# The last stage's output products with the weight as stationary operand and 512 tokens moving, in a fused recurrence and feed-forward kernel on one Trainium2 core

## The chip, the cores and the metric

The kernel runs on one core of a Trainium2 chip. The metric is the device time of one execution in microseconds (us), the median over several runs. The core's engines are called as the profile calls them: PE is TensorE (matrix products), PEld its weight loads, DVE is VectorE, ACT is ScalarE, POOL is GpSimd, and SP is the engine whose queue issues the DMAs.

## The reference

Three parts follow each other: a linear recurrence with decay over 768 positions (2 batches, 8 heads of 48), a mixture of four experts on the 1,536 tokens, and a last feed-forward stage. Only the last is touched:

```python
def _moe2_ref(x, w_in, w_out) -> np.ndarray:      # x 1536 x 384, w_in 384 x 2048, w_out 2048 x 384
    h = x @ w_in
    g = h * (1.0 / (1.0 + np.exp(-1.702 * h)))
    return (g @ w_out).astype(np.float32)
```

## The kernel before, in words

All activations between the parts are kept on the chip with the 384 model features as rows, in three tiles of 128 partitions (`KT` = 3), and the tokens as columns. Every product is made three times to keep float32 precision: an operand is split into a high part that the PE reads exactly and a low remainder, and high x high, high x low and low x high are added up in PSUM (`PASSES`). So each logical product of 128 x 128 x columns is three matmuls.

The expert part and the last stage are one list of steps. A step j is 128 hidden features of one stage for one block of tokens (512 tokens; the first four blocks of expert 0 have 256). `hidden(j)` (L909) makes these 128 hidden features: three k-tiles by three passes, nine matmuls with the input weight stationary and the tokens of `x_hi` or `x_lo` moving. `output(j)` multiplies the hidden features by the output weight and adds to the block's output in PSUM. In the expert part (L931) that is also nine matmuls: for each of three tiles of 128 output features, the weight is stationary and the tokens of `h_hi` or `h_lo` move. In the last stage (L946) it is turned round: for each of four tiles of 128 tokens (`t`), the hidden features are stationary and the 384 columns of the output weight move, so that the output has its tokens as rows, as the reference wants it. That is twelve matmuls.

The last stage has 48 steps: three blocks of 512 tokens, 16 steps each (`STEPS1` is the number of the first). PE's order is written out: hidden(j), then output(j-2), from the third step of the stage on; at the end the last two outputs stand behind each other. Between hidden and output of a step ACT and DVE work in turns: ACT takes the sigmoid of the hidden features (L581, into `acc`), DVE multiplies (L740), ACT rounds the result to the high part `h_hi` (L583), DVE makes the low part `h_lo` (L742). `hidden(j)` waits until the hidden bank of step j-2 was read, `output(j)` waits for `h_lo` of its step. ACT waits for the outputs of step j-3 before it overwrites its slot of `h_hi` (a ring of three).

The finished outputs of a block are copied out of PSUM by ACT (`store_block`, L562), one copy for each tile of 128 tokens. In ACT's order they come before the sigmoid of the block's step 18 (two steps into the next block), and for the last block at the very end. A copy waits for the semaphore `tile`, which PE raises after each of a block's last products but the final one, and for `l2` for the final one; the copies go into `out_sb`, a ring of `OUT_RING` pieces in the tensor `p_bc`, and SP stores each to the output in DRAM (L412) as it is done. The PSUM banks of the outputs are two sets of three (`OUT_SETS`, 0 to 2 and 5 to 7); four token tiles a block walk through both sets (`out_bank2`).

Of the kernel before, what the change touches and what calls it, by code (L numbers as in the profile page):

```python
# [31 lines left out]
F32 = mybir.dt.float32  # L32
F32R = mybir.dt.float32r
U32 = mybir.dt.uint32
ACT = mybir.ActivationFunctionType

P = 128
# [3 lines left out]
N = B * S  # L41
DM = H * D
# [5 lines left out]
KT = DM // P  # L48
NB = 512
BLOCKS = N // NB  # L50
# [9 lines left out]
MOE_BLOCKS = len(SPANS)  # L60
# [6 lines left out]
SCALED = [64, 32, 16, 8, 4, 2]  # L67
XBUF = 3
HRING = 3
OUT_RING = 4  # L70
MID = P // 2
W_LEAST, W_MOST = 0.5, 1.5
AT_RING = 3
# [4 lines left out]
def build(nc, rkT, rkvN, w_rows, w_flat, u_flat, probs, weights, out):  # L78
    p_dram = nc.dram_tensor("p_normalised", [E, N], F32, kind="Internal").ap()
    ctx = ExitStack()  # L80
    with ctx:
# [10 lines left out]
        sem = {}  # L92
# [11 lines left out]
        s_prob = [ctx.enter_context(nc.semaphore(f"s_prob{i}")) for i in range(2)]  # L104
        s_store = [ctx.enter_context(nc.semaphore(f"s_store{i}")) for i in range(OUT_RING)]

        def sb(stack, name, shape, dt=F32):
            return stack.enter_context(nc.sbuf_tensor(name, shape, dt))
# [7 lines left out]
        bank = ctx.enter_context(nc.psum_tensor("bank", [P, 8, 512], F32))  # L116
# [13 lines left out]
        p_bc = [sb(ctx, "p_bc0", [P, N]), None]  # L130
# [41 lines left out]
        sig = [acc[:, 0, 0:NB], acc[:, 1, 0:NB]]  # L172
        gated = [acc[:, 2, 0:NB], acc[:, 0, NB:2 * NB]]

        out_sb = [p_bc[0][:, i * DM:(i + 1) * DM] for i in range(OUT_RING)]


        w_row, w_ok = part[0:1, 0, 0:H * D], part[0:1, 1, 0:H * D]
# [12 lines left out]
        OUT_SETS = ((0, 1, 2), (5, 6, 7))  # L191

        def out_tile(n, k):


            if n < SMALLS:
                return bank[:, 5 + k // 2, k % 2 * SMALL:(k % 2 + 1) * SMALL]
            return bank[:, OUT_SETS[n % 2][k], :]

        def out_bank2(m):  # L200

            return OUT_SETS[m // KT % 2][m % KT]

        def spans(ap, m):

# [10 lines left out]
        def where(j):  # L216

            if j < STEPS1:
                n, f = divmod(j, FT)
                t, size = SPANS[n]  # L220
                return expert_of(n), f, slice(t, t + size), f == 0, f == FT - 1
            b, f = divmod(j - STEPS1, F2 // P)
            return E + f // FT, f % FT, slice(b * NB, (b + 1) * NB), f == 0, f == F2 // P - 1
# [20 lines left out]
        def part_of(tensors, f, piece):  # L244
            t = tensors[piece]
            if piece:
                return t[:, f * DM:(f + 1) * DM]
            return t[:, :].rearrange("p (k n) -> p k n", k=KT)[:, :, f * P:(f + 1) * P]
# [44 lines left out]
        def _(sp):  # L293
# [9 lines left out]
            def load_stage(s):  # L303
                for i in range(2):
                    sp.dma_start(staging[i][:, :], weights[2 * s + i]).then_inc(s_stage[i], 16)
# [101 lines left out]
                load_stage(e + 1)  # L407
            sp.wait_ge(sem["wlo"], 2 * FT * E)
            load_stage(STAGES - 1)
            for n in range(BLOCKS * NB // P):  # L410
                sp.wait_ge(sem["ev2"], n + 1)
                sp.dma_start(out[n * P:(n + 1) * P, :], out_sb[n % OUT_RING]).then_inc(s_store[n % OUT_RING], 16)  # L412
            for i in range(OUT_RING):
                sp.wait_ge(s_store[i], 16 * (BLOCKS * NB // P // OUT_RING))


        @block.gpsimd
# [91 lines left out]
        def _(act):  # L509
# [40 lines left out]

            def store_block(b):

                for t in range(NB // P):
                    m = b * (NB // P) + t

                    if t < NB // P - 1:
                        act.wait_ge(sem["tile"], b * (NB // P - 1) + t + 1)
                    else:
                        act.wait_ge(sem["l2"], STEPS1 + (b + 1) * F2 // P)
                    if m >= OUT_RING:  # L560
                        act.wait_ge(s_store[m % OUT_RING], 16 * (m // OUT_RING))
                    act.activation(out_sb[m % OUT_RING], bank[:, out_bank2(m), 0:DM], ACT.Copy).then_inc(sem["ev2"], 1)  # L562

            def step(j):
                g = j - STEPS1
# [56 lines left out]
            with act.Else():  # L622
                for u in range(UNITS):
                    c, p = divmod(u, PAIRS)
# [20 lines left out]
            for j in range(JOIN, STEPS):  # L645
                step(j)
            store_block(BLOCKS - 1)


# [221 lines left out]
        def _(pe):  # L871
            pe.wait_ge(sem["ident"], 2)
            pe.wait_ge(sem["wr"], 1)
            for p in range(PAIRS):
                last = pe.transpose(table_t[:, p * P:(p + 1) * P], w_rev[:, p, :], ident[:, :])
# [4 lines left out]
            xs, hs = (x_hi, x_lo), (h_hi, h_lo)  # L880
# [3 lines left out]
            def wait_weights(s, f, piece):  # L884
                if s == 0:
                    pe.wait_ge(sem["wlo0"], STAGE0.index((f, piece)) + 1)
                else:
                    pe.wait_ge(sem["wlo"], 2 * FT * (s - 1) + 2 * f + piece + 1)
# [25 lines left out]
            def output(j):  # L914

                s, f, tokens, first, last_f = where(j)
                size = tokens.stop - tokens.start
                slot = j % HRING
                if tokens.start == 0:
                    wait_weights(s, f, 1)  # L920
                pe.wait_ge(sem["hlo"], j + 1)
                if j < STEPS1:
                    n = j // FT
                    if first and 1 <= n < SMALLS:
                        pe.wait_ge(sem["ev1"], KT * n)
                    if first and n > SMALLS:
                        pe.wait_ge(sem["ev1"], KT * (n - 1))
                    for k in range(KT):
                        for i, (a, c) in enumerate(PASSES):
                            w = part_of(w_parts[a][s % 2], f, 1)  # L930
                            last = pe.matmul(out_tile(n, k), w[:, k * P:(k + 1) * P], hs[c][:, slot, 0:size],  # L931


                                             start=(first and i == 0 and not (n < SMALLS and k == 1)),
                                             stop=(last_f and i == 2 and (n >= SMALLS or k > 0)))
                else:
                    for t in range(NB // P):
                        m = tokens.start // P + t
                        if first:
                            if m < 2 * KT:  # L940
                                pe.wait_ge(sem["ev1"], KT * (MOE_BLOCKS - 2) + m + 1)
                            else:
                                pe.wait_ge(sem["ev2"], m - 2 * KT + 1)
                        for i, (a, c) in enumerate(PASSES):
                            w = part_of(w_parts[a][s % 2], f, 1)
                            last = pe.matmul(bank[:, out_bank2(m), 0:DM], hs[c][:, slot, t * P:(t + 1) * P], w,  # L946
                                             start=(first and i == 0), stop=(last_f and i == 2))
                        if last_f and t < NB // P - 1:
                            last.then_inc(sem["tile"], 1)
                last.then_inc(sem["l2"], 1)  # L950

# [2 lines left out]
            with pe.If(quick == 1):  # L954
# [46 lines left out]
                for what, i in SCHEDULE:  # L1001
                    if what == "unit":
                        unit(i)
                    elif what == "weigh":
                        weigh(i)
                    elif what == "hidden":
                        hidden(i)
                    elif what == "output":
                        output(i)
            with pe.Else():  # L1010
                def level(dst, col, g, m, p, c):

                    rows = slice(g * HP, (g + 1) * HP)
                    x, o = c % XBUF, c % 2
                    width = 64 if m == 64 else P
                    if m == 1:
                        key, rec = k_in[rows, x, p, :], r_in[rows, x, p, 1:P:2]
                    else:
                        n = SCALED.index(m)
                        key, rec = G["k_lev"][rows, o, n, p, 0:width], G["r_lev"][rows, o, n, p, :]  # L1020
                    return pe.matmul(dst[0:width, g, col:col + HP], key, rec, start=True, stop=True)
# [20 lines left out]
                for u in range(UNITS):  # L1042
                    c, p = divmod(u, PAIRS)
# [8 lines left out]
                    for n, m in enumerate(HIGH):  # L1052
                        for g in range(2):
                            last = level(G_HIGH, n * HP, g, m, p, c)
# [3 lines left out]
                    for n, m in enumerate(LOW):  # L1058
                        for g in range(2):
                            last = level(G_LOW, n * HP, g, m, p, c)  # L1060
                    last.then_inc(sem["g_low"], 1)
                    if ci < CPB - 1:
                        if updates(u) > 1:
                            pe.wait_ge(sem["g_st"], updates(u) - 1)
                        for g in range(2):
                            last = pe.matmul(G_KV[LIVE[g], 0:D], kn_in[:, c % XBUF, (2 * p + g) * D:(2 * p + g + 1) * D],
                                             v_in[:, c % XBUF, 2 * p + g, :], start=True, stop=True)
# [5 lines left out]
                for what, i in GENERAL:  # L1073
                    if what == "hidden":
                        hidden(i)
                    elif what == "output":
                        output(i)
            for j in range(JOIN, STEPS):
                hidden(j)
                if j <= STEPS1:  # L1080
                    output(j - 1)
                if j >= STEPS1 + 2:
                    output(j - 2)
# [51 lines left out]
```

## Time and profile before

| | us |
|---|---|
| median of 3 runs | 704.76 |
| lowest and highest | 704.3, 707.44 |
| span of the profiled execution, first to last instruction | 702.7 |
| PE busy | 682.2 (97%) |
| DVE, ACT, POOL busy | 240.9, 215.4, 180.0 |
| last stage, first output matmul (504.92) to the last matmul's end (699.75) | 194.8 |

For the profiled execution the span is known and not its device time; the median lies 2.1 us above the span. Busy time of PE counts a matmul from its start to its modelled end, and these overlap (a matmul is shown with 0.33 to 0.40 us and the next one starts 0.17 to 0.23 us behind it), so what a matmul costs in a stream is read from start to start.

### The profile page before, as it was taken

The numbers are of one execution on the slowest core, as the hardware profiler recorded it, in microseconds if no ns is written. First come the engines' busy times: TensorE is split into PE (matmuls) and PEld (weight loads), VectorE is DVE, ScalarE is ACT, GpSimd is POOL, SyncE is SP. The second block draws the span as 40 slices with busy tenths as digits, with TensorE's granted clock in tenths as the row PEclk, the third lists the DMA queues.
The fourth block names the chain that finished last, engine by engine and source line by source line (L and its number), as shares of the span: only waits on it lengthen the run. The fifth ranks groups of instructions, "written<-read, shape, count | busy, mean of one in ns | idle before, by whom it ended". The sixth has DMA issues, their size and how long they took to land.

```text
span 702.7 us, 9199 instructions
## 1 busy us (share of the span) xinstructions
PE 682.2 (97%) x3636; PEld 563.4 (80%) x3636; DVE 240.9 (34%) x433; ACT 215.4 (31%) x455; POOL 180.0 (26%) x172
## 2 busy tenths in 40 slices
PE   3899999999999999999999999999999999999998
PEld 1457778778888888888888888888899999999997
DVE  7666755432131212121213223121443333333332
ACT  4245532332332221122221122322453232323223
POOL 5424242200532423032422043532292000000000
PEclk9999999999999999999999999999999999999999
DMA  7253462101032004010004000021000010001001
GB/s 278 83 209 128 132 250 72 65 5 52 1 122 104 0 1 165 15 46 0 1 1 179 1 1 0 1 105 75 0 1 1 1 46 0 1 1 45 1 1 45
DMA packets 11987, 39.24 MB, mean 56 GB/s; under 512 B 3233, under 2 KB 6050, under 8 KB 10658
## 3 DMA queue, kind: packets, MB, share of 16 engines
q1 hardware_dynamic: 11938, 38.60, 15.1%
q8 instruction: 30, 0.49, 0.3%
q14 instruction: 19, 0.16, 0.1%
HBM read 35.61 MB, written 2.38 MB: 54 GB/s over the span
## 4 chain that ended last, share of the span: by engine, by line
PE 95%; DVE 3%; issue 1%; ACT 0%; DMA 0%; DVEq 0%
PE bank L909 42%; PE bank L931 28%; PE bank L946 14%; PE bank L984 3%; PE bank L970 2%; PE bank L967 2%; PE bank L993 1%; DVE q_r_mid L760 1%; DVE q_k_mid L757 1%; DVE q_a_t L768 0%; DVE q_tab_k L661 0%; DMA w_sb<-w_rows 0%; DVE w_pow L656 0%; DVE psum_sb L685 0%; DVE psum_sb L687 0%
## 5 line engine op out<-in xcount | busy, mean ns | idle before, releaser
L909 PE MATMUL bank<-x_hi,w_hi 128*128 128x512 f32 (+1 forms) x480 | 178.2, 371 | 1.5 <-issue 1.5
L909 PE MATMUL bank<-x_hi,w_lo 128*128 128x512 f32 (+1 forms) x480 | 177.8, 370 | 0.0
L909 PE MATMUL bank<-x_lo,w_hi 128*128 128x512 f32 (+1 forms) x480 | 177.7, 370 | 0.0
L732 DVE SCALAR_TENSOR_TENSOR h_lo<-bank,h_hi 128x512 fp32r<-128x512 f32 (+1 forms) x112 | 68.9, 615 | 295.6 <-ACT h_hi L575 295.6
L575 ACT ACTIVATE h_hi<-bank 128x512 fp32r<-128x512 f32 (+1 forms) x112 | 60.1, 537 | 314.0 <-PE bank L909 314.0
L485 POOL TENSOR_TENSOR w_lo<-staging,w_hi 128x384 fp32r<-128x384 f32 x80 | 82.1, 1038 | 174.3 <-ACT w_hi L537 174.3
L931 PE MATMUL bank<-h_hi,w_hi 128*128 128x512 f32 (+1 forms) x336 | 123.0, 366 | 1.3 <-DVE acc L722 1.3
L931 PE MATMUL bank<-h_lo,w_hi 128*128 128x512 f32 (+1 forms) x336 | 120.4, 358 | 0.0
L931 PE MATMUL bank<-h_hi,w_lo 128*128 128x512 f32 (+1 forms) x336 | 120.4, 358 | 0.0
L909 PEld LDWEIGHTS bank<-x_hi,w_hi 128*128 128x128 f32 x480 | 90.8, 189 | 17.5 <-issue 3.3
L909 PEld LDWEIGHTS bank<-x_hi,w_lo 128*128 128x128 f32 x480 | 90.8, 189 | 15.1
L909 PEld LDWEIGHTS bank<-x_lo,w_hi 128*128 128x128 f32 x480 | 90.8, 189 | 14.0
L931 PEld LDWEIGHTS bank<-h_hi,w_hi 128*128 128x128 f32 x336 | 63.1, 188 | 15.3 <-issue 5.2
L931 PEld LDWEIGHTS bank<-h_lo,w_hi 128*128 128x128 f32 x336 | 63.2, 188 | 9.5
L931 PEld LDWEIGHTS bank<-h_hi,w_lo 128*128 128x128 f32 x336 | 63.2, 188 | 9.3
L740 DVE TENSOR_TENSOR acc<-bank,acc 128x512 f32<-128x512 f32 x48 | 33.2, 692 | 94.7 <-ACT acc L581 94.7
L946 PE MATMUL bank<-w_lo,h_hi 128*128 128x384 f32 x192 | 64.8, 337 | 0.0
L946 PE MATMUL bank<-w_hi,h_hi 128*128 128x384 f32 x192 | 64.6, 337 | 0.0
L946 PE MATMUL bank<-w_hi,h_lo 128*128 128x384 f32 x192 | 64.5, 336 | 0.0
L581 ACT ACTIVATE acc<-bank 128x512 f32<-128x512 f32 x48 | 28.6, 596 | 89.1 <-PE bank L909 89.1
L494 POOL TENSOR_TENSOR acc<-acc,part 128x512 f32<-128x512 f32 x27 | 34.2, 1293 | 84.9 <-DVE part L722 84.9
L537 ACT ACTIVATE w_hi<-staging 128x384 fp32r<-128x384 f32 x96 | 47.4, 515 | 0.9 <-DMA staging<-weights 0.9
(67 smaller groups left out, 553.3 us busy)
## 6 DMA issues: line engine op xcount, KB each, us to landing
staging<-weights SPq DMA_DIRECT2D x10, 1536.0 KB, 8.6
rkv_in<-rkv_n SPq DMA_DIRECT2D x12, 576.0 KB, 4.6
rk_in<-rk_t SPq DMA_DIRECT2D x12, 512.0 KB, 3.8
staging<-weights SPq DMA_DIRECT2D x4, 768.0 KB, 8.9
p_bc<-p_normalised SPq DMA_DIRECT2D x4, 768.0 KB, 5.1
out<-p_bc SPq DMA_DIRECT2D x12, 192.0 KB, 2.0
y_sb<-y_sb SPq DMA_DIRECT2D x72, 8.0 KB, 1.8
u_bc<-u_flat SPq DMA_DIRECT2D x1, 192.0 KB, 6.0
```

The lines of the kernel that those rows point to most:

```text
L485: pool.tensor_tensor(part_of(w_lo[s % 2], f, piece), part_of(staging, f, piece), part_of(w_hi[s % 2], f, piece).bitcast(F32), ALU.subtract ...
L494: pool.tensor_tensor(acc[:, k, cols], acc[:, k, cols], part[:, i % 2, :], ALU.add).then_inc(sem["acc"], 1)
L537: act.activation(part_of(w_hi[s % 2], f, piece), part_of(staging, f, piece), ACT.Copy).then_inc(sem["whi"], 1)
L575: act.activation(h_hi[:, j % HRING, 0:size], hid, ACT.Relu).then_inc(sem["hhi"], 1)
L581: act.activation(sig[g % 2], hid, ACT.Sigmoid, scale=1.702).then_inc(sem["sig"], 1)
L732: dve.scalar_tensor_tensor(h_lo[:, slot, 0:size], hid, 0.0, h_hi[:, slot, 0:size].bitcast(F32), ALU.max, ALU.subtract).then_inc(sem["hlo"], 1)
L740: dve.tensor_tensor(gated[g % 2], hid, sig[g % 2], ALU.mult).then_inc(sem["gate"], 1)
L909: last = pe.matmul(bank[:, HID[j % 2], 0:tokens.stop - tokens.start], w[:, k, :], xs[c][:, k, tokens], start=(n == 0), stop=(n == 3 * KT - 1))
L931: last = pe.matmul(out_tile(n, k), w[:, k * P:(k + 1) * P], hs[c][:, slot, 0:size],   start=(first and i == 0 and not (n < SMALLS and k == ...
L946: last = pe.matmul(bank[:, out_bank2(m), 0:DM], hs[c][:, slot, t * P:(t + 1) * P], w, start=(first and i == 0), stop=(last_f and i == 2))
L967: pe.matmul(y_of(Y_BANK, g, p), state[rows, ci % 2, p, :], r_in[rows, x, p, :], start=True, stop=False)
L984: pe.matmul(bank[:, A_BANKS[u % 2], 0:2 * P], k_mid[:, o, p, :], r_mid[:, o, p, :, :], start=True, stop=True).then_inc(sem["q_a"], 1)
```

## The change

The output products of the last stage take the form of the expert part. For each of three tiles of 128 output features (`k`) the weight's 128 columns are stationary and all 512 tokens of `h_hi` or `h_lo` move, nine matmuls a step instead of twelve. The output of a block lies in one set of three banks, features as rows, 512 tokens as columns. `store_block` makes three copies of 128x512 instead of four of 128x384, SP issues nine stores of 256 KB instead of twelve of 192 KB, each into 128 rows of 2,048 bytes of an output tensor that is 384 x 1,536. The ring `out_sb` has three pieces of 512 columns instead of four of 384, so each copy from the second block on also waits for the store of one block before. The final transposition is made on the host.

```diff
-OUT_RING = 4
+OUT_RING = 3
+STORES = BLOCKS * KT
-        out_sb = [p_bc[0][:, i * DM:(i + 1) * DM] for i in range(OUT_RING)]
+        out_sb = [p_bc[0][:, i * NB:(i + 1) * NB] for i in range(OUT_RING)]
-            for n in range(BLOCKS * NB // P):
-                sp.wait_ge(sem["ev2"], n + 1)
-                sp.dma_start(out[n * P:(n + 1) * P, :], out_sb[n % OUT_RING]).then_inc(s_store[n % OUT_RING], 16)
+            for m in range(STORES):
+                b, k = divmod(m, KT)
+                sp.wait_ge(sem["ev2"], m + 1)
+                sp.dma_start(out[k * P:(k + 1) * P, b * NB:(b + 1) * NB], out_sb[m % OUT_RING]).then_inc(s_store[m % OUT_RING], 16)
 def store_block(b):
-                for t in range(NB // P):
-                    m = b * (NB // P) + t
-                    if t < NB // P - 1:
-                        act.wait_ge(sem["tile"], b * (NB // P - 1) + t + 1)
+                for k in range(KT):
+                    m = b * KT + k
+                    if k < KT - 1:
+                        act.wait_ge(sem["tile"], b * (KT - 1) + k + 1)
...
-                    act.activation(out_sb[m % OUT_RING], bank[:, out_bank2(m), 0:DM], ACT.Copy).then_inc(sem["ev2"], 1)
+                    act.activation(out_sb[m % OUT_RING], out_tile(MOE_BLOCKS + b, k), ACT.Copy).then_inc(sem["ev2"], 1)
 def output(j):
-                    for t in range(NB // P):
-                        m = tokens.start // P + t
+                    b = tokens.start // NB
+                    for k in range(KT):
+                        m = b * KT + k
...
-                            last = pe.matmul(bank[:, out_bank2(m), 0:DM], hs[c][:, slot, t * P:(t + 1) * P], w,
+                            last = pe.matmul(out_tile(MOE_BLOCKS + b, k), w[:, k * P:(k + 1) * P], hs[c][:, slot, :],
                                              start=(first and i == 0), stop=(last_f and i == 2))
-    out = nc.dram_tensor("out", (N, DM), F32, kind="ExternalOutput").ap()
+    out = nc.dram_tensor("out", (DM, N), F32, kind="ExternalOutput").ap()
-    return result.results[0]["out"]
+    return np.ascontiguousarray(result.results[0]["out"].T)
```

On PE, between two hidden steps of the last stage, this stood before (in a name pair the moving operand is named first for a product with a stationary weight; `w_hi,h_hi` has the weight moving):

```order
3128 L946 MATMUL bank<-w_hi,h_hi 128x384
3129 L946 MATMUL bank<-w_hi,h_lo 128x384
3130 L946 MATMUL bank<-w_lo,h_hi 128x384
3131 L946 MATMUL bank<-w_hi,h_hi 128x384
3132 L946 MATMUL bank<-w_hi,h_lo 128x384
3133 L946 MATMUL bank<-w_lo,h_hi 128x384
3134 L946 MATMUL bank<-w_hi,h_hi 128x384
3135 L946 MATMUL bank<-w_hi,h_lo 128x384
3136 L946 MATMUL bank<-w_lo,h_hi 128x384
3137 L946 MATMUL bank<-w_hi,h_hi 128x384
3138 L946 MATMUL bank<-w_hi,h_lo 128x384
3139 L946 MATMUL bank<-w_lo,h_hi 128x384
```

And on PE at the same kind of place now, with the first matmul of the next hidden step behind it (line 945 is the changed line 946, line 907 the unchanged 909):

```order
3137 L945 MATMUL bank<-h_hi,w_hi 128x512
3138 L945 MATMUL bank<-h_lo,w_hi 128x512
3139 L945 MATMUL bank<-h_hi,w_lo 128x512
3140 L945 MATMUL bank<-h_hi,w_hi 128x512
3141 L945 MATMUL bank<-h_lo,w_hi 128x512
3142 L945 MATMUL bank<-h_hi,w_lo 128x512
3143 L945 MATMUL bank<-h_hi,w_hi 128x512
3144 L945 MATMUL bank<-h_lo,w_hi 128x512
3145 L945 MATMUL bank<-h_hi,w_lo 128x512
3146 L907 MATMUL bank<-x_hi,w_hi 128x512
```

Twelve matmuls of 384 columns have become nine of 512, the same number of columns; the place in PE's order is the same.

On ACT, at the end of the program, this stood before (L581 and L583 are the sigmoid and the rounding of the last step, L562 the copies of the last block):

```order
532 L581 ACTIVATE acc<-bank 128x512
533 L583 ACTIVATE h_hi<-acc 128x512
534 L581 ACTIVATE acc<-bank 128x512
535 L583 ACTIVATE h_hi<-acc 128x512
536 L562 ACTIVATE p_bc<-bank 128x384 x4
```

And on ACT at the same place now:

```order
532 L579 ACTIVATE acc<-bank 128x512
533 L581 ACTIVATE h_hi<-acc 128x512
534 L579 ACTIVATE acc<-bank 128x512
535 L581 ACTIVATE h_hi<-acc 128x512
536 L560 ACTIVATE p_bc<-bank 128x512 x3
```

Four copies of 384 columns have become three of 512, at the same place.

## Rows read from the trace of the kernel before

**Rows 1.** The page: busy time, then granted clock over 40 slices, then the chain.

```profile
PE 682.2 (97%) x3636; PEld 563.4 (80%) x3636; DVE 240.9 (34%) x433; ACT 215.4 (31%) x455; POOL 180.0 (26%) x172
...
PEclk9999999999999999999999999999999999999999
...
PE 95%; DVE 3%; issue 1%; ACT 0%; DMA 0%; DVEq 0%
```

**Rows 2.** Two stretches: length, then busy us of PE, PEld, DVE, ACT, POOL.

```profile
300.00:400.00 100.00, 100.00 (x443) 82.79 (x442) 22.87 (x34) 20.97 (x40) 27.52 (x25) 1.00 0.11 40
513.29:597.05 83.76, 83.76 (x422) 75.90 (x421) 30.33 (x41) 30.50 (x55) 18.09 (x17) 1.00 0.03 10
```

**Rows 3.** The chain in order of time, from 492: start, us, what.

```profile
498.96 2.04 PE bank L931 x9
501.00 4.08 PE bank L909 x18
```

**Rows 4.** The same view, from 480 to the end.

```profile
509.27 2.10 PE bank L946 x12
511.37 2.08 PE bank L909 x9
...
693.48 6.28 PE bank L946 x36
```

**Rows 5.** Timeline of PE around the first last-stage output: start, duration, instruction.

```profile
504.92 0.33 PE L946 MATMUL bank<-w_hi,h_hi 128*128 128x384 f32 x1
...
505.44 0.35 PE L946 MATMUL bank<-w_hi,h_hi 128*128 128x384 f32 x1
505.63 0.34 PE L946 MATMUL bank<-w_hi,h_lo 128*128 128x384 f32 x1
505.80 0.34 PE L946 MATMUL bank<-w_lo,h_hi 128*128 128x384 f32 x1
505.99 0.33 PE L946 MATMUL bank<-w_hi,h_hi 128*128 128x384 f32 x1
...
507.02 0.39 PE L909 MATMUL bank<-x_hi,w_hi 128*128 128x512 f32 x1
```

**Rows 6.** Timeline of PE in the last output steps and of ACT beside them.

```profile
694.38 0.33 PE L946 MATMUL bank<-w_hi,h_hi 128*128 128x384 f32 x1
...
695.60 0.69 DVE L742 TENSOR_TENSOR h_lo<-acc,h_hi 128x512 fp32r<-128x512 f32 x1 [0.70 <-ACT h_hi L583]
...
699.41 0.34 PE L946 MATMUL bank<-w_lo,h_hi 128*128 128x384 f32 x1
```

**Rows 7.** Timeline of one step: ACT and DVE between two hidden steps.

```profile
689.13 0.33 PE L946 MATMUL bank<-w_hi,h_hi 128*128 128x384 f32 x1
...
689.33 0.60 ACT L581 ACTIVATE acc<-bank 128x512 f32<-128x512 f32 x1 [2.14 <-PE bank L909]
...
691.41 0.69 DVE L742 TENSOR_TENSOR h_lo<-acc,h_hi 128x512 fp32r<-128x512 f32 x1 [0.70 <-ACT h_hi L583]
```

**Rows 8.** Timeline of ACT at a block's end, then the waits from 495 on.

```profile
569.87 1.61 ACT L562 ACTIVATE p_bc<-bank 128x384 f32<-128x384 f32 x4
...
ACT acc L581 <- PE bank L909: 89.1, 45, 2.2
```

**Rows 9.** Groups of ACT from 500 on: busy us, mean ns, idle before.

```profile
L581 ACT ACTIVATE acc<-bank 128x512 f32<-128x512 f32 x47 | 28.0, 596 | 86.9 <-PE bank L909 86.9
...
L562 ACT ACTIVATE p_bc<-bank 128x384 f32<-128x384 f32 x12 | 5.2, 490 | 2.7 <-PE bank L946 2.7
```

**Rows 10.** The last instructions of ACT (chain, from 690), and the DMA issues of the page.

```profile
699.79 0.49 ACT p_bc L562
...
staging<-weights SPq DMA_DIRECT2D x10, 1536.0 KB, 8.6
...
rk_in<-rk_t SPq DMA_DIRECT2D x12, 512.0 KB, 3.8
...
out<-p_bc SPq DMA_DIRECT2D x12, 192.0 KB, 2.0
```

More of the change, by code:

```diff
@@ L198, in out_tile @@
             return bank[:, OUT_SETS[n % 2][k], :]
-        def out_bank2(m):
-            return OUT_SETS[m // KT % 2][m % KT]
         def spans(ap, m):
@@ L409, in _ @@
             load_stage(STAGES - 1)
-            for n in range(BLOCKS * NB // P):
-                sp.wait_ge(sem["ev2"], n + 1)
-                sp.dma_start(out[n * P:(n + 1) * P, :], out_sb[n % OUT_RING]).then_inc(s_store[n % OUT_RING], 16)
+            for m in range(STORES):
+                b, k = divmod(m, KT)
+                sp.wait_ge(sem["ev2"], m + 1)
+                sp.dma_start(out[k * P:(k + 1) * P, b * NB:(b + 1) * NB], out_sb[m % OUT_RING]).then_inc(s_store[m % OUT_RING], 16)
             for i in range(OUT_RING):
-                sp.wait_ge(s_store[i], 16 * (BLOCKS * NB // P // OUT_RING))
+                sp.wait_ge(s_store[i], 16 * (STORES // OUT_RING))
         @block.gpsimd
@@ L945, in output @@
                             w = part_of(w_parts[a][s % 2], f, 1)
-                            last = pe.matmul(bank[:, out_bank2(m), 0:DM], hs[c][:, slot, t * P:(t + 1) * P], w,
+                            last = pe.matmul(out_tile(MOE_BLOCKS + b, k), w[:, k * P:(k + 1) * P], hs[c][:, slot, :],
                                              start=(first and i == 0), stop=(last_f and i == 2))
-                        if last_f and t < NB // P - 1:
+                        if last_f and k < KT - 1:
                             last.then_inc(sem["tile"], 1)
```

## The prediction

> **What bounds the kernel now.** I read the page first: PE is busy 97% of the span, the chain that ended last is PE for 95% of it, and the granted clock is full (2.4 GHz) in all 40 slices [rows 1]. DVE, ACT and POOL are each busy for about a third. Next the stretches: in the last stage, 513.29 to 597.05, PE is busy for all 83.76 us, so it waits for nobody, while DVE and ACT are busy for 30 us each [rows 2]. The time of this stage is therefore the number of matmuls times the distance from one start to the next, and nothing else. The reader should look for that distance, not for the duration: durations overlap.
>
> It is read from the chain in order of time. The nine expert output matmuls with 512 moving columns take 2.04 us, and the 18 hidden matmuls at the seam of the stages take 4.08 us: 0.2267 us each in both cases [rows 3]. In the last stage twelve matmuls of 384 columns take 2.10 us, and the nine hidden ones of 512 columns, which took 2.04 before, take 2.08 [rows 4]. A step of the last stage is 4.19 us (513.29 to 597.05 are 20 steps: 83.76 / 20 = 4.188 [rows 2]). A step of the expert part is 4.08 us.
>
> **The matmuls: what a width costs.** Both kinds of step stream the same number of columns through PE: 12 x 384 = 9 x 512 = 4,608, which is 1.920 us at 2.4 GHz. So the change removes no column. It removes three matmuls, and what it earns is what a matmul costs beyond its columns. Two rows give that. Undisturbed, 29 matmuls of 384 columns run from 694.38 to 699.41, 0.1734 us each [rows 6]: columns are 0.1600, the rest is 13.4 ns. For 512 columns it is 0.2267 - 0.2133 = 13.4 ns [rows 3]. The same surcharge at both widths, so it is paid per matmul: three fewer are 0.040 us a step, over 48 steps 1.9 us.
>
> The second piece is larger. Twelve undisturbed matmuls would be 12 x 0.1734 = 2.08 us, but the block takes 2.10, and the hidden block beside it 2.08 where the same instructions took 2.04 [rows 3, 4]. The timeline shows where: the first six matmuls after the change of width, 504.92 to 505.99, take 1.07 us instead of 1.04, one of them 0.19 (505.44 to 505.63), and the next six take 1.03, the undisturbed pace [rows 5]. The same is seen in every step, and the nine hidden ones after the narrow ones are too slow together by 0.04. The cause is not shown by a wait, since there is none. What ties it to the change of width: the 18 hidden matmuls at 501.00, already last stage, with 512 in front and behind, run at 0.2267 [rows 3]; the narrow ones at the end, from the seventh after a change on, run at 0.1734 while DVE still writes `h_lo` beside them [rows 6]. So it is neither the stage nor the neighbours' work in general. With the change no width changes any more: all matmuls from 504.92 on are 128x512, in the form that the expert part runs at 0.2267 (443 matmuls in 100 us [rows 2]).
>
> The sum, from the first last-stage output at 504.92 (nothing before it changes). From there PE has 48 outputs and 45 hidden steps: 93 x 2.04 = 189.72 us, so the last matmul's turn ends at 694.64, its start is 694.41. Before, its start was 699.41 [rows 6]. So PE is through **5.0 us** earlier (5.00 by the starts).
>
> The rows of this case show 13.4 ns at two widths and 0.06 us lost at the changes [rows 3 to 6], and by them I go. The Trainium skill, TensorE: Matmul & The Clock Gate, section "Back-to-back issue gap", speaks against the gain: it gives for an isolated matmul the columns at 2.4 GHz plus 2.5 ns. By that figure, as an estimate, three fewer matmuls would be 7.5 ns a step and 0.4 us in all; the trace doesn't agree with it.
>
> **PE's partners.** In a step the sigmoid (L581) starts 0.2 us after the hidden matmuls end, and the low part (L742) is there 2.97 us after that end (689.13 to 691.41 + 0.69) [rows 7]. It is needed by output two steps later, over 6 us after; a step 0.11 us shorter takes nothing from this that counts. ACT waited 89.1 us for PE's hidden products in all [rows 8], about 2 us a step. If that cover were gone, a step would cost what ACT and DVE need, 2.97 us, still below 4.08. Loads are not touched: POOL's splitting and the weight transfers end before they are needed by many steps, and the trace shows PE busy throughout [rows 2].
>
> **The copies.** A copy of 384 columns takes 0.49 us, a PSUM read of 512 columns by ACT (the sigmoid) 0.60 [rows 9]. At a block's end before, four copies took 1.61 us back to back [rows 8]; now three take 3 x 0.60 = 1.8 at most. They sit in ACT's order before the sigmoid two steps into the next block, and ACT has 2 us of idle time a step, so at the two inner block ends this is free either way. What queues behind the copies is that sigmoid, and PE's hidden step two later; that is covered by the same slack. The new wait of each copy for a store of the block before: that store was issued 16 steps, 65 us, earlier and lands in 2 us [rows 10], so it costs nothing. The banks: each block now keeps to one set of three and the next one has the other, so no output waits for a copy just made.
>
> At the very end the last copy is on the path. It starts behind the last matmul (699.79, ended 700.28 [rows 10]). Now the matmul's own end is later after its start by 0.39 - 0.34 = 0.05 us [rows 5, 6], and the copy is longer by **0.11** (0.60 - 0.49). The copy of the tile before it has 3 x 0.2267 = 0.68 us until the last tile is ready and needs 0.60, so it is out of the way.
>
> **The stores.** Nine of 256 KB for twelve of 192 KB, and only the last is on the path. 192 KB land in 2.0 us, 512 KB (a load) in 3.8 [rows 10]. A line through both is 1.8 / 320 = 5.6 ns per KB, so 64 KB more are at most 0.36 us; the lower bound is 0, if the landing is a fixed time. Stores are nearest to the store's own row and part of the 2.0 is fixed; I take **0.15**. The rows in DRAM are 2,048 bytes with gaps between them, where before they lay close; no row shows a store with gaps, so I bound it by the same two ends and, in the last rival, by much more.
>
> **The sum.** -5.00 + 0.05 + 0.11 + 0.15 = -4.69 us. On the profiled execution: 702.7 - 4.7 = 698.0 span. The median was 2.06 above that span; with the same around it, 704.76 - 4.69 = **700.1 us**, 0.67% less. About 0.5%, 3.5 us, is what a measurement of this kernel can tell from no change, so the forecast is beyond it, but by little more than 1 us.
>
> **Rivals.** *First, the loss at the changes of width stays*, because it belongs to something else in the last stage (reads of `h` as an operand beside ACT and DVE). Then only the per-matmul part comes: 0.04 x 48 = 1.92, less 0.31 at the end, 703.1 us. If the hidden matmuls alone stay at 2.08, it is (4.19 - 4.12) x 48 = 3.3, less 0.31: 701.8. For it speaks that I can name no mechanism; against it speak the undisturbed 18 hidden matmuls inside the stage [rows 3].
> *Second, the change doesn't do what it says*: excluded for the matmuls by the order shown, nine by 128x512 a step.
> *Third, only columns count*: nine wide output matmuls take the 2.10 us of the twelve narrow ones and the hidden ones keep their 2.08 [rows 4]. Then PE gains nothing and the end costs 0.31: 705.1 us, no change. It wants 0.233 us for a matmul of 512 columns with `h` moving, where the expert part shows 0.2267 for that very form [rows 3], so it has little for it. (The small surcharge in the Trainium skill's TensorE: Matmul & The Clock Gate would come out here too; no row of this trace has a surcharge that small.)
> *Fourth, slower: the last store.* If a store with gaps between its rows lands as late as the largest loads, 8.6 us [rows 10] instead of 2.0, it costs 6.6 us at the end against 4.8 earned: 706.6 us. It decides from a landing of 2.0 + 4.8 = 6.8 us on. Against it: 2,048 bytes a row are more than the 1,536 before, and there is the same number of rows per store.
>
> **How the numbers follow.** The forecast has 0.84. The first rival 0.09, the third 0.04, the fourth 0.03. The forecast's own range is 699.3 to 701.2: the store's bounds are -0.15 and +0.2, and medians of a few runs of the kernel before lay between 704.3 and 707.44, so the upper side gets more. To the overall range I add the milder form of the first rival: 699.3 to 702.2. Faster by over 0.5% (below 701.2): the forecast but for its upper edge, 0.79. Within 0.5%: the first and third rival and that edge, 0.17. Slower: 0.04.
>
> **What the profile after would show.** Nine last-stage output matmuls in 2.04 us in the chain, and the hidden ones between them also 2.04, not 2.08; if these stay at 2.08, the first rival holds. PE busy throughout the stage. The last matmul starting near 694.4, the last copy of 0.60 us, the span's end near 698.0; store issues of 256 KB landing in 2.0 to 2.4 us. The prediction is wrong if the 512-column products show more than 0.2267 each, if PE has idle time at the two inner block ends, or if the landing of the last store is over 3 us.

## The result and the profile after

The changed kernel takes 699.51 us (median of 20 runs, 692.99 to 702.73), the kernel before 704.8 in the same session (20 runs, 697.81 to 707.76). The ratio is 0.992 with a 95% interval of 0.9898 to 0.9942: faster, by 0.6 to 1.0%. (The quotient of the two medians, 0.9925, is not quite the same.) Applied to the 704.76 us that the forecast started from, 0.992 is 699.1 us, 1.0 us less than forecast and 0.2 us below the low end of the stated range (699.3). The miss is small beside the noise: the interval, applied in the same way, goes from 697.6 to 700.7 us and holds the forecast of 700.1, and the median of 699.51 itself lies inside the range.

The profiled execution has a span of 698.7 us. The first view is the chain in order of time (start, us, what), first at the seam to the last stage and then at its end; it answers to [rows 3, 4, 10]. L907 are the hidden products, L945 the last stage's output products, L560 the copies.

```profile
499.69 2.04 PE bank L929 x9
501.73 4.08 PE bank L907 x18
505.81 2.04 PE bank L945 x9
507.85 2.04 PE bank L907 x9
...
689.41 6.13 PE bank L945 x27
695.54 0.02 issue
695.56 0.60 ACT p_bc L560
```

Nine output products take 2.04 us where twelve took 2.10 [rows 4], and the unchanged hidden products between them take 2.04 where they took 2.08. In the stretch 513 to 595 PE is never idle, as before [rows 2]:

```profile
513.00:595.00 82.00, 82.00 (x364) 67.94 (x363) 30.48 (x41) 31.48 (x56) 19.11 (x18) 1.00 0.03 10
```

In the timeline of PE the first output product of the last stage starts at 505.64 and the last one at 695.14:

```profile
505.64 0.39 PE L945 MATMUL bank<-h_hi,w_hi 128*128 128x512 f32 x1
...
695.14 0.39 PE L945 MATMUL bank<-h_hi,w_lo 128*128 128x512 f32 x1
```

That is 189.50 us, against 699.41 - 504.92 = 194.49 before [rows 5, 6]: 4.99 less. The stage begins 0.72 us later than in the profile of before, though nothing ahead of it was changed. Of the stores the page says the following, against 192 KB and 2.0 us before [rows 10]:

```profile
out<-p_bc SPq DMA_DIRECT2D x9, 256.0 KB, 2.1
```

### The profile page after: what moved, and what is told of

Same layout as the page of the kernel before. It is cut to its first block, busy times and chain, and to the rows that moved or that the text cites. A ratio compares the mean times of both kernels' runs of the same rounds, so it can differ in the third digit from the quotient of the medians.

```text
span 698.7 us, 8902 instructions
## 1 busy us (share of the span) xinstructions
PE 676.7 (97%) x3492; PEld 543.6 (78%) x3492; DVE 242.3 (35%) x433; ACT 215.2 (31%) x452; POOL 179.8 (26%) x172
## 4 chain that ended last, share of the span: by engine, by line
PE 94%; DVE 4%; issue 1%; ACT 0%; DMA 0%; DVEq 0%
PE bank L907 42%; PE bank L929 29%; PE bank L945 14%; PE bank L983 3%; PE bank L969 2%; PE bank L966 2%; DVE q_r_mid L758 1%; PE bank L992 1%; DVE q_k_mid L755 1%; DVE q_a_t L766 0%; DMA w_sb<-w_rows 0%; DVE q_tab_k L659 0%; DVE w_pow L654 0%; DVE psum_sb L683 0%; DVE psum_sb L685 0%
## 5 line engine op out<-in xcount | busy, mean ns | idle before, releaser
L907 PE MATMUL bank<-x_hi,w_hi 128*128 128x512 f32 (+1 forms) x480 | 178.4, 372 | 1.4 <-issue 1.4
L907 PE MATMUL bank<-x_lo,w_hi 128*128 128x512 f32 (+1 forms) x480 | 177.1, 369 | 0.0
L907 PE MATMUL bank<-x_hi,w_lo 128*128 128x512 f32 (+1 forms) x480 | 177.0, 369 | 0.0
L907 PEld LDWEIGHTS bank<-x_hi,w_hi 128*128 128x128 f32 x480 | 90.9, 189 | 18.7 <-issue 3.3
L907 PEld LDWEIGHTS bank<-x_hi,w_lo 128*128 128x128 f32 x480 | 90.9, 189 | 15.0
L907 PEld LDWEIGHTS bank<-x_lo,w_hi 128*128 128x128 f32 x480 | 90.9, 189 | 14.8
L945 PE MATMUL bank<-h_lo,w_hi 128*128 128x512 f32 x144 | 56.1, 389 | 0.0
L945 PE MATMUL bank<-h_hi,w_lo 128*128 128x512 f32 x144 | 56.1, 389 | 0.0
L945 PE MATMUL bank<-h_hi,w_hi 128*128 128x512 f32 x144 | 56.1, 389 | 0.0
```

Of the source, the lines that this page charges most:

```text
L907: last = pe.matmul(bank[:, HID[j % 2], 0:tokens.stop - tokens.start], w[:, k, :], xs[c][:, k, tokens], start=(n == 0), stop=(n == 3 * KT - 1))
L945: last = pe.matmul(out_tile(MOE_BLOCKS + b, k), w[:, k * P:(k + 1) * P], hs[c][:, slot, :], start=(first and i == 0), stop=(last_f and i = ...
```

## The experiments

Two questions were open. Inside the last stage: is the loss of 0.07 us a step really a matter of changing widths (theory W), or of which operand is stationary (theory S), or of the neighbours ACT and DVE? And for the whole: where do the 0.6 to 0.9 us come from by which the measured times (5.3 us between the medians, 5.6 by the ratio) went beyond the stage's 4.7? For e1 to e4 one execution each was timed, beside one of the kernel before (699.96 us); their profiles are read, and their times say little.

**e1, the hidden features stationary again, but 512 columns moving.**

```diff
-                    wait_weights(s, f, 1)
+                    wait_weights(s, 1 if j >= STEPS1 and f == 0 else f, 1)
...
-                            w = part_of(w_parts[a][s % 2], f, 1)
-                            last = pe.matmul(out_tile(MOE_BLOCKS + b, k), w[:, k * P:(k + 1) * P], hs[c][:, slot, :],
+                            o = max(0, (f + 1) * DM - NB)
+                            last = pe.matmul(out_tile(MOE_BLOCKS + b, k), hs[c][:, slot, k * P:(k + 1) * P], w_parts[a][s % 2][1][:, o:o + NB],
```

> The changed kernel, but the hidden features are stationary again and 512 columns of the output weight move (the 384 of the step and 128 of a neighbouring one), nine matmuls a step. The output is not the reference's: its last product is left out in this form and a meaningless one of the same size is made. Theory W (the loss of 0.07 us a step in the kernel before comes from alternating 512 and 384 columns): output and hidden blocks of 2.04 us each, every matmul 0.227 us, a step of 4.08. Theory S (it comes from having the hidden features as the stationary operand): the hidden blocks stay at 2.08, the output blocks above 2.04, a step of 4.11 to 4.15.

The chain in the middle of the stage:

```profile
532.66 2.04 PE bank L945 x9
534.70 2.04 PE bank L907 x9
```

Both blocks take 2.04 us: no loss, with the hidden features as stationary operand. Theory S falls, as W expected. (The one run took 694.99 us. That is not the work of this edit; the part ahead of the last stage was quick, as is told below.)

**e2, the weight stationary, but twelve products of 384 tokens.**

```diff
-                    for k in range(KT):
+                    for t, k in enumerate((0, 0, 1, 2)):
-                            last = pe.matmul(out_tile(MOE_BLOCKS + b, k), w[:, k * P:(k + 1) * P], hs[c][:, slot, :],
+                            last = pe.matmul(out_tile(MOE_BLOCKS + b, k)[:, 0:DM], w[:, k * P:(k + 1) * P], hs[c][:, slot, 0:DM],
...
```

> The changed kernel, weight stationary, but twelve matmuls of 384 tokens a step instead of nine of 512 (the first tile is made twice, the last 128 tokens of each block are left out, so the output is not the reference's). Theory W: as in the kernel before, twelve in 2.10 us with the first six too slow by 0.03 together, hidden blocks 2.08, a step of 4.19. Theory S: no loss, twelve in 2.08 and hidden blocks in 2.04, a step of 4.12.

The chain in the middle of the stage, and the timeline of PE at the change to the narrow form:

```profile
533.45 2.08 PE bank L907 x9
535.53 2.10 PE bank L945 x12
...
535.37 0.33 PE L945 MATMUL bank<-h_hi,w_hi 128*128 128x384 f32 x1
...
535.90 0.35 PE L945 MATMUL bank<-h_hi,w_hi 128*128 128x384 f32 x1
536.08 0.34 PE L945 MATMUL bank<-h_lo,w_hi 128*128 128x384 f32 x1
...
536.44 0.33 PE L945 MATMUL bank<-h_hi,w_hi 128*128 128x384 f32 x1
```

The loss is back in full, 2.10 and 2.08, and the first products after the change are the ones that lose: the first six take 1.07 us (535.37 to 536.44), as in the kernel before [rows 5], and the fourth is again shown with 0.35 us instead of 0.33. Averaged over the 45 such blocks of a trace, the fourth distance is 0.185 us in both kernels and the largest. Which operand is stationary makes no difference; the width does. (The one run took 702.25 us.)

**e3, each output product cut into two of 256 tokens.**

```diff
-                            last = pe.matmul(out_tile(MOE_BLOCKS + b, k), w[:, k * P:(k + 1) * P], hs[c][:, slot, :],
-                                             start=(first and i == 0), stop=(last_f and i == 2))
+                            for c0 in (0, SMALL):
+                                last = pe.matmul(out_tile(MOE_BLOCKS + b, k)[:, c0:c0 + SMALL], w[:, k * P:(k + 1) * P],
+                                                 hs[c][:, slot, c0:c0 + SMALL],
+                                                 start=(first and i == 0 and c0 == 0), stop=(last_f and i == 2 and c0 > 0))
```

> The changed kernel with each output matmul cut into two of 256 tokens: 18 a step, the same columns, the same output. A surcharge of 13.4 ns per matmul gives 18 x 0.120 = 2.16 us; with theory W a further loss at the changes of width, the hidden blocks between 2.04 and 2.10, a step of 4.22 to 4.30. If only columns counted, the output blocks would stay at 2.04 and the step at 4.08.

```profile
533.62 2.15 PE bank L946 x18
535.78 2.07 PE bank L907 x9
```

The surcharge per product holds at a third width: 18 x (0.1067 + 0.0134) = 2.16 us, measured 2.15. A step is 4.22 us where the changed kernel has 4.08, for the same columns. The loss at the changes is there too, but smaller: 0.03 us in the hidden block and none in the narrow one. Each of these products has its own weight load, as in all kernels here (the pages count as many PEld as PE instructions), so whether the surcharge belongs to the product or to its weight load was not separated. (The one run took 701.46 us.)

**e4, the kernel before with its order in pairs**, so that the width changes half as often. (The start of the loop, with the first two steps of the stage, is left out here.)

```diff
...
-                if j >= STEPS1 + 2:
-                    output(j - 2)
+            for j in range(STEPS1 + 2, STEPS, 2):
+                hidden(j)
+                hidden(j + 1)
+                output(j - 2)
+                output(j - 1)
```

> The kernel before, with PE's order in the last stage in pairs: hidden, hidden, output, output, so that the width changes half as often. Same work and output. Theory W with a loss per change: two steps take 8.24 + 0.07 = 8.31 us instead of 8.375, so 4.155 a step, and the stage is 1.6 us shorter. Theory S or a loss caused by ACT and DVE beside PE: 4.19 a step as before. PE idle anywhere in the stage would mean that the pairs made a new wait and the run tells nothing.

```profile
524.98 4.18 PE bank L946 x24
529.16 4.12 PE bank L909 x18
```

Two steps take 8.30 us, W's number (8.31) and not 8.375. The loss is paid once per change, not per product: 18 wide ones in 4.12 are 0.04 over 4.08, just what nine lost before. A loss caused by the neighbours ACT and DVE would have stayed at 0.07 us a step, since their work is the same. The pairs made one new wait at the start of the stage, between two hidden steps:

```profile
505.51 0.39 PE L909 MATMUL bank<-x_hi,w_lo 128*128 128x512 f32 x1
506.04 0.47 PE L909 MATMUL bank<-x_hi,w_hi 128*128 128x512 f32 x1
506.35 0.40 PE L909 MATMUL bank<-x_lo,w_hi 128*128 128x512 f32 x1
```

The two distances are 0.84 us together instead of 0.45, so it cost 0.39 us, once. The expectation had said that an idle PE anywhere in the stage would void the run. That was stricter than needed: no other distance between two products of the stage is above 0.25 us, and the pairs behind this place can be read. The sum agrees: from the last expert product to the last product of all it is 699.12 - 501.43 = 197.69 us, against 699.41 - 500.61 = 198.80 before. That is 1.11 less, and 1.50 without the new wait, where 1.6 was expected. The run took 704.37 us.

**e5 and e6, the changed kernel again and the kernel before against itself**, five rounds each.

> The changed kernel once more, unchanged, beside the kernel before. My theory: the change is worth 4.7 us (ratio 0.9933) whatever the run, and the rest of what was measured (0.992, 5.6 us) is variation of the first 200 us, which both kernels share. Then the ratio lies between 0.990 and 0.996, the part from the first last-stage output matmul to the last is 189.5 us again to within 0.02, and the start of that part moves by some tenths or more from profile to profile. The rival, that the change also shortens something ahead of the last stage, wants a ratio of 0.992 or less again and a start earlier than 504.9.

> The kernel before, timed against itself: the null case. It shows how far a ratio of medians moves with nothing changed. If the variation between executions explains the distance between 0.992 and 0.9933, the ratio here is 1 within 0.003, with single runs spread over 8 to 10 us as before, and the profiled execution has its first last-stage output matmul at another time than 504.92 but the stage itself unchanged, 194.5 us from the first to the last start.

e5 gave 699.8 us against 704.17, ratio 0.9933 (0.9897 to 0.9969). That is the forecast ratio to the last digit, and with such an interval it is luck; the medians are 4.4 us apart. e6 gave 703.94 against 704.17, ratio 0.9988 (0.9955 to 1.0022). So with nothing changed, a ratio of this kernel moves by a tenth of a per cent and its interval is a third of a per cent to each side. In the timelines of PE these are the first and the last output product of the last stage of e5:

```profile
506.64 0.39 PE L945 MATMUL bank<-h_hi,w_hi 128*128 128x512 f32 x1
...
696.14 0.39 PE L945 MATMUL bank<-h_hi,w_lo 128*128 128x512 f32 x1
```

It starts 1.00 us later than in the first profile after the change, and the stage from there to the last start is again 189.50 us (506.64 to 696.14). In e6, the kernel before, they are

```profile
504.19 0.33 PE L946 MATMUL bank<-w_hi,h_hi 128*128 128x384 f32 x1
...
698.68 0.34 PE L946 MATMUL bank<-w_lo,h_hi 128*128 128x384 f32 x1
```

with 194.49 us between them. The stage repeats to 0.01 us; what moves between executions lies ahead of it. That both profiles of the changed kernel start the stage later than those of the kernel before also speaks against a gain ahead of it.

**What moves ahead of it.** In e1 the last stage started at 499.86, 5.8 us before that of the first profile after the change (505.64), so its recurrence was compared with the others. The group of the 128x256 product of each recurrence unit, in the stretch 26 to 34 us, first the kernel before, then e1 (columns: busy us, mean ns, idle before), and behind them the stretch 20 to 50 us of before, e6 and e1 (granted clock is the third number from the end):

```profile
L984 PE MATMUL bank<-q_r_mid,q_k_mid 128*128 128x256 f32 x7 | 4.3, 703 | 0.0
...
L983 PE MATMUL bank<-q_r_mid,q_k_mid 128*128 128x256 f32 x11 | 4.0, 436 | 0.0
...
20.00:50.00 30.00, 27.85 (x149) 14.01 (x149) 16.42 (x43) 11.86 (x33) 11.06 (x11) 1.00 0.47 157
20.00:50.00 30.00, 27.77 (x151) 13.84 (x151) 16.80 (x43) 12.15 (x33) 11.15 (x11) 0.55 0.48 162
20.00:50.00 30.00, 25.39 (x214) 14.42 (x215) 23.72 (x57) 15.31 (x42) 12.26 (x11) 0.94 0.61 205
```

A product takes 703 ns in the kernel before and 436 in e1, and PE gets 214 products done in these 30 us instead of 149. e6 shows products as long (703 to 715 ns) beside a granted clock of 0.55, that is 1.2 GHz for most of the stretch; e1 has 0.94. The 1.00 in the row of the kernel before can't be right for this stretch: its products are as long and as few as those of e6. By the durations, five of the eight profiles so far, those of the two kernels, e4, e5 and e6, run the recurrence at half clock until about 50 us, but for a moment near 22 us in e6. e1, e2 and e3 run it at full clock from 26 to 27 us, and of these e2 and e3 are back at half for a part of the time between 39 and 48 (e2 has 0.72 there, e3 0.81, e1 1.00). All eight have the same work there. Over the two kernels' runs in the first session, e5 and e6, the changed kernel had 6 of 32 executions at 693.0 to 695.1 us and the others at 698.9 to 704.1, and the kernel before 8 of 55 at 697.7 to 699.4 and the others at 703.3 to 709.5. The gap of some 4 us between the groups is the same in both. The next four runs tested whether the clock of the recurrence makes it.

Two smaller things move as well. The first product of the recurrence starts between 9.30 us (e1) and 11.11 (the first profile after the change), in both kernels. And PE waits once behind a product that starts between 162 and 171 us, 1.6 to 2.1 us from this start to the next; in e1, e5, e7 and e8 the clock is at half for a few microseconds behind this wait, in the other eight profiles it is not. The stretch 170 to 175 us of e5 and of e6:

```profile
170.00:175.00 5.00, 3.63 (x13) 3.05 (x14) 0.00 (x0) 0.58 (x2) 0.00 (x0) 0.77 0.03 8
170.00:175.00 5.00, 4.51 (x24) 3.97 (x25) 1.49 (x4) 1.42 (x3) 1.10 (x2) 1.00 0.03 7
```

In e5 the products of 512 columns there start 0.43 us apart instead of 0.23 (172.90, 173.32, 173.75). Up to the 201st hidden product e5 is 0.40 us behind e6 (140.32 against 139.92), and from the 401st on (221.95 against 219.50) 2.45 us, as at the start of the last stage. So the longer wait and the fallen clock cost 2.05 us. What decides how either place comes out was not tried.

**e7 and e8, extra matmuls at the start.** In e7 two 128x512 products run behind the four transposes, where PE was idle; e8 has four smaller ones more in the waits of the first units (the last line below, e8 alone). Theory C is that the clock of the recurrence separates the groups of times.

```diff
+            def warm(n, pairs):
+                for _ in range(n):
+                    pe.matmul(bank[:, HID[0], 0:pairs * P], ident[:, :], w_rev[:, 0:pairs, :], start=True, stop=True)
+            warm(2, PAIRS)
...
+                    warm({0: 1, 1: 1, 3: 2}.get(u, 0), 2)
```

> The changed kernel with two extra 128x512 matmuls of real table data between the four transposes at the start and PE's first wait (5.8 to about 9.2 us, where PE stood idle); their result is overwritten before anyone reads it. In the profiles so far the recurrence runs at half clock until 50 us in most executions (a unit takes 2.7 us) and at full clock from 19 us in the quick ones (1.56 us a unit), and these end 6 us earlier. Theory C (the level of the clock in the recurrence is what separates the groups of times): if the extra work raises the clock before 20 us, the time is 692 to 695 in most executions, ratio 0.983 to 0.987. Rival: two matmuls so early don't carry over to the recurrence, the time is that of the changed kernel, 699.5, ratio 0.9933, or up to 0.5 us more if they delay the first unit.

> As the run before, and four more extra matmuls of 256 columns in the waits of the first units (one each behind units 0 and 1, two behind unit 3, where PE waited 1.0, 0.7 and 2.5 us). Theory C: the clock is raised by 15 us and stays, the time is 692 to 695 in nearly all executions, ratio 0.983 to 0.987, and the spread over executions shrinks from 10 us to 3. Rival: the extra matmuls only delay the units they stand before, by up to 0.3 us each, and the ratio is 0.993 to 0.995.

e7 split evenly: 693.3, 693.3, 699.88 and 701.52 us, ratio 0.9884 (0.9803 to 0.9966), between what the two theories expected. Its profile is of the execution of 701.52. The first two products of the recurrence after the extra work take 0.67 us, the next two 1.22:

```profile
10.00 0.67 PE L988 MATMUL bank<-q_r_mid,q_k_mid 128*128 128x256 f32 x2 [1.40 <-DVE q_r_mid L758]
...
13.77 1.22 PE L988 MATMUL bank<-q_r_mid,q_k_mid 128*128 128x256 f32 x2 [1.19 <-DVE q_r_mid L758]
...
10.00:20.00 10.00, 6.19 (x28) 2.85 (x28) 8.95 (x14) 2.55 (x8) 7.09 (x7) 0.56 0.72 269
20.00:50.00 30.00, 27.86 (x153) 14.05 (x153) 16.42 (x43) 11.87 (x33) 11.09 (x11) 0.52 0.48 157
```

So the clock rose and fell again. e8 gave 692.85 us, 691.74 to 696.07, ratio 0.984 (0.9774 to 0.9906), and its profile, of the execution of 696.07, has 0.90 for 20 to 50 us. It is at full clock later than expected, though: the products at 24.90 still take 1.22 us, and those at 26.99 take 0.70. The times come out as theory C has them. Four runs of e7 are too few to say how often two products are enough; with the waits filled all five were below 697 us.

**e9 and e10, the kernel before with the same extra matmuls, and e8 once more**, side by side.

> The kernel before (twelve matmuls of 384 columns in the last stage) with the same extra matmuls at the start as in e8. Theory C: it goes to 696 to 699 us in most executions, ratio to the kernel before 0.990 to 0.993, since the gain of the quick front has nothing to do with the form of the last stage. Rival: the quick front of e8 was chance or needs the changed kernel, ratio 0.997 to 1.0.

> The kernel of e8 once more, beside e9. With the front alike in both, the difference between the two medians is the last stage alone: 4.7 us by my theory, so 692 to 694 us here, ratio 0.983 to 0.986, against 697 to 698.5 for e9. If the difference is 5.6 us or more, the change earned more than the last stage shows.

e9 gave 697.36 us (10 runs, ratio 0.9911, 0.9877 to 0.9945), inside what theory C expected. e10 gave 693.05 (6 runs, 0.9811 to 0.9914); its time is as expected and its ratio, 0.9863, a little above the 0.983 to 0.986. The stretch 20 to 50 us of e9 and of e10:

```profile
20.00:50.00 30.00, 25.73 (x216) 15.08 (x217) 23.79 (x58) 15.29 (x43) 12.45 (x12) 0.94 0.62 206
20.00:50.00 30.00, 25.16 (x210) 14.71 (x208) 23.57 (x57) 14.92 (x42) 12.43 (x12) 0.94 0.61 206
```

Both fronts are quick now, with more than 200 products instead of 149; the products are short from 17.7 us on in e9 and from 22.2 in e10. The extra matmuls give the kernel before 704.42 - 697.36 = 7.1 us and the changed one 6.5 to 6.8 (from its 699.51 and 699.8 in other sessions). So the gain belongs to the front and not to the form of the last stage. The distance between the two forms is 697.36 - 693.05 = 4.3 us, against 4.6 by the traces, as is worked out below, and well under the 5.6 that would have meant a gain elsewhere. The kernel of e8 and e10 is the best measured, 693 us. The spread of 3 us expected for e8 was not reached: its five runs span 4.3 us, and one of e10's six took 699.73.

## Why the prediction was right in its steps and missed its range

*PE's part*: forecast -5.00, measured -4.99. Width per product 0.2267, hidden blocks back at 2.04, PE busy throughout: each as put. None of the three signs by which the prediction would have been wrong was seen. That the loss belonged to the change of width was inferred from 18 undisturbed products and a settled tail; e1, e2 and e4 show it.

*The end*: the copy takes 0.60 us as forecast. From the copy's end to the span's end it was 2.43 us (700.28 to 702.71) and is 2.56 (696.16 to 698.72), so the store costs 0.13 where 0.15 was put. The 64 KB more and the gaps between the rows cost this much together, and the fourth rival falls.

*The copies at the inner block ends*: free, as put. (The wait for the store of one block before is not new, as the prediction calls it: four copies a block and a ring of four had the same wait.) ACT still waits for PE behind them:

```profile
569.47 1.08 ACT L560 ACTIVATE p_bc<-bank 128x512 f32<-128x512 f32 x2
571.12 0.60 ACT L579 ACTIVATE acc<-bank 128x512 f32<-128x512 f32 x1 [0.58 <-PE bank L907]
```

*The sum*: from the first last-stage product to the end of the span it was 702.71 - 504.92 = 197.79 us and is 698.72 - 505.64 = 193.08. That is -4.71, forecast -4.69. One term was left out. The prediction put the time outside the span at 2.06 us, "with the same around it", by taking the span of one execution from the median of others. The record has time and span of every execution: the distance is 1.89 to 1.98 us (mean 1.94) in the 23 of the kernel before beside e5, and 2.09 on average in the 20 of the changed kernel in the first session. So the change costs another 0.15 us outside the span, for a reason that no run shows, and a device time 4.6 us lower is what the traces give. This goes the other way from the miss.

*The rivals*: the first (the loss stays) fell with 2.08 becoming 2.04; the third (only columns count) with a surcharge of 13.3 to 13.4 ns at 256, 384 and 512 columns. The Trainium skill, TensorE: Matmul & The Clock Gate, "Back-to-back issue gap", has 2.5 ns for this on isolated matmuls; these streams don't agree with it.

*What failed* is the lower edge of the range, in the step "How the numbers follow", and not the mechanism. The edge, 699.3, lies 0.8 us below the forecast. The store's bound is 0.15 of that; for the rest there is no row, only three single times of the kernel before (704.3, 704.76 and 707.44, which the prediction calls medians). So the variation of what surrounds the last stage was put at next to nothing on the lower side, although the prediction itself names 3.5 us as what a measurement of this kernel can tell from no change. More runs of the kernel before reach down to 697.7 us, and the ratio's interval is 1.6 us to each side. The same kernel's median was 704.8, 704.17, 703.94, 703.98 and 704.42 in five measurements. For the same change the medians were 5.3 us apart in the first session and 4.4 in e5, and e6 moved by 0.2 with no change at all.

Where the excess of the first session, 1.0 us over the forecast, comes from is open. The last stage doesn't hold it: that part repeats to 0.01 us. The quick recurrence alone doesn't explain it either. Without the quick executions the medians of the first session are 705.3 and 700.1 us, 5.2 apart, and those beside e5 still 4.4 apart. It is rather the upper side that differs: 9 of the 20 executions of the kernel before were at 705.3 or more in the first session, and none of the 12 of e6. The later first product and the fallen clock at 170 us are of the right size for that, but no execution of the upper group of the kernel before was profiled.

The first paragraph of the prediction has a related error: it took the clock row of the page, full in all 40 slices, at its word [rows 1]. For the last stage that is true (products of 512 columns start 0.2267 us apart there, and 0.43 where the clock is at half), for 10 to 50 us it is not, and the durations of the recurrence's products would have told. Two expectations have a smaller one: e7's says that the quick executions are at full clock from 19 us, and the profiles up to then show it to stay there from 26 us; e8's had it raised by 15 us and staying.

## What to carry to other kernels

Where PE never waits, cost an edit by the distance from one start to the next and not by columns: each matmul with its weight load carries a fixed surcharge (here 13.4 ns at 2.4 GHz, in float32 split form), and each change between two widths costs some more (0.07 us for a pair of changes between 384 and 512), also on matmuls that the edit doesn't touch. So give neighbouring streams one width, the widest, or at least group them. Before a range is written, look at whether the executions of the kernel fall into groups, make the range no narrower than a repeated measurement moves, and check the clock by the durations of like instructions. When the clock of an early stretch decides between the groups, extra matmuls in PE's early waits can be worth more than the edit under study (here 6.5 to 7.1 us against 4.6).

## What the runs showed of the hardware that was not expected

The loss after a change of width is the same to a nanosecond in every step and in different kernels, and it fades. Averaged over the blocks of a trace, the first six products of 384 columns behind 512 lose 0.026 us together and those from the seventh on nothing; nine of 512 behind 384 lose 0.041, and in e4, where 18 stand there, the tenth and later ones lose nothing. Behind 256 columns only the first five of 512 lose, 0.027. What in PE makes it was not tried and stays open.

PE's clock can stay at half through 30 us in which PE is busy for 27.8 of them, here with products of 48 to 256 columns, and be at full for much of the same work in another execution. PE at full clock was then busy for less of the time (25.4 us of 30), and the stretch was done sooner. In e7 two matmuls of 512 columns ahead raised it for a moment only in the profiled execution; with four more in the first waits it was up from 26 us in e8, 22 in e10 and 18 in e9, but for short falls (e9's hidden products of 256 columns take 391 to 416 ns between 32 and 40 us, e10's 281 to 307). Why it is up in one execution and not in another, with the same instructions, is open. And the clock record of a trace can say full where the durations say half.
